# A three-stage attention and MLP kernel: 32x32 block transposes on the vector engine, and weighted sums as 32x64 tiles

## The reference

```python
batch, n_heads, seq, head_dim = (4, 8, 768, 64)
chunk, left_ctx, right_ctx = (32, 16, 8)
...
for c in range(seq // chunk):
    k_full = concatenate([mem_k, k[l_start:r_end]])      # 8 + 56 = 64 rows
    scores = scale * matmul(q_c, k_full.T)
    a = exp(scores - max(scores)); a = a / (sum(a) + 1e-09)
    out[c_start:c_end] = matmul(a, v_full)
...
h = maximum(maximum(x @ w1, x @ w2), x @ w3); x = h @ w_out      # 3072 x 512, d_ff 768
h = x @ w_in; g = where(h >= 1, h, where(h <= -1, 0, (h + 1) ** 2 / 4)); out = g @ w_out   # d_ff 2048
```

## Time and profile before

| what | value |
|---|---|
| median of 3 runs | 988.83 us (988.78 to 989.06) |
| the profiled execution, its own time | 989.49 us |
| its span, first to last instruction | 987.7 us |
| PE busy | 970.1 us (98%), 7968 matmul records |
| DVE busy | 469.3 us (48%) |
| ACT busy | 354.6 us (36%) |
| POOL busy | 150.1 us (15%) |

### The profile page before, as it was taken

How to read it: one execution, slowest core, us unless ns; L and a number is a source line. 1 busy time by engine, 2 the same in 40 slices (tenths; PEclk the granted TensorE clock), 3 DMA queues, 4 the chain that set the end, 5 groups by cost and what they waited for, 6 DMA issues and landing times.

```text
span 987.7 us, 18546 instructions
## 1 busy us (share of the span) xinstructions
PE 970.1 (98%) x7968; PEld 905.5 (92%) x7968; DVE 469.3 (48%) x713; ACT 354.6 (36%) x553; POOL 150.1 (15%) x176
## 2 busy tenths in 40 slices
PE   5999999999999999999999999999999999999998
PEld 4999999999999999999988989899898989888887
DVE  4572514344252433425356655566545665454452
ACT  3341222222122222222344535544455544444253
POOL 1112342315225231000000000000000000000000
PEclk9999999999999999999999999999999999999999
DMA  9452743745464461042635565655657545574532
GB/s 371 174 204 97 261 178 129 251 142 181 176 226 174 167 229 61 1 171 64 248 136 196 204 250 192 224 192 192 240 192 251 189 162 192 189 255 173 194 117 107
DMA packets 32206, 181.52 MB, mean 184 GB/s; under 512 B 3456, under 2 KB 7552, under 8 KB 21888
## 3 DMA queue, kind: packets, MB, share of 16 engines
q0 software_dynamic: 9216, 92.28, 26.7%
q1 hardware_dynamic: 22912, 88.09, 24.2%
HBM read 144.70 MB, written 35.65 MB: 183 GB/s over the span
## 4 chain that ended last, share of the span: by engine, by line
PE 97%; ACT 1%; DVE 1%; DMA 0%; issue 0%
PE mlp L465 23%; PE mlp L466 23%; PE mlp L467 22%; PE attn_ps L467 3%; PE attn_ps L466 3%; PE attn_ps L465 3%; PE scores_ps L467 3%; PE scores_ps L466 3%; PE scores_ps L465 3%; PE attn_ps L458 3%; PE scores_ps L434 2%; PE trans_ps L467 1%; PE trans_ps L466 1%; PE trans_ps L465 1%; PE trans_ps L441 1%; DMA qk_raw<-qk_l 0%
## 5 line engine op out<-in xcount | busy, mean ns | idle before, releaser
L465 PE MATMUL mlp<-x_hi,w_hi 128*128 128x384 f32 x576 | 197.4, 343 | 1.6 <-issue 1.6
L467 PE MATMUL mlp<-x_lo,w_hi 128*128 128x384 f32 x576 | 193.7, 336 | 0.0
L466 PE MATMUL mlp<-x_hi,w_lo 128*128 128x384 f32 x576 | 193.4, 336 | 0.0
L465 PE MATMUL mlp<-yc,wi 128*128 128x384 f32 x448 | 149.6, 334 | 1.5 <-ACT up L628 1.5
L466 PE MATMUL mlp<-yc,wi 128*128 128x384 f32 x448 | 150.8, 337 | 0.0
L467 PE MATMUL mlp<-yc,wi 128*128 128x384 f32 x448 | 149.7, 334 | 0.0
L743 ACT ACTIVATE ramp<-up,half_col 128x768 f32<-128x768 f32 x64 | 60.1, 939 | 197.0 <-DVE up L959 177.9
L465 PEld LDWEIGHTS mlp<-x_hi,w_hi 128*128 128x128 f32 x576 | 108.7, 189 | 3.6 <-issue 1.7
L466 PEld LDWEIGHTS mlp<-x_hi,w_lo 128*128 128x128 f32 x576 | 108.8, 189 | 0.0
L467 PEld LDWEIGHTS mlp<-x_lo,w_hi 128*128 128x128 f32 x576 | 108.7, 189 | 0.0
L465 PEld LDWEIGHTS mlp<-yc,wi 128*128 128x128 f32 x448 | 84.1, 188 | 9.6 <-ACT up L628 1.8
(11 more groups left out here) (111 smaller groups left out, 1643.7 us busy)
## 6 DMA issues: line engine op xcount, KB each, us to landing
wi<-wi_scratch POOLq DMA_DIRECT2D x32, 1792.0 KB, 7.5
wo<-wo_scratch POOLq DMA_DIRECT2D x32, 1024.0 KB, 5.1
qk_raw<-qk_l SPq DMA_DIRECT2D x24, 768.0 KB, 8.3
wi_scratch<-stage_a SPq DMA_DIRECT2D x8, 1792.0 KB, 8.8
v_raw<-v_l SPq DMA_DIRECT2D x24, 512.0 KB, 4.8
wo_scratch<-stage_a SPq DMA_DIRECT2D x8, 1024.0 KB, 6.8
y_scratch<-y_stage SPq DMA_DIRECT2D x32, 192.0 KB, 3.2
y_raw<-y_scratch SPq DMA_DIRECT2D x8, 768.0 KB, 5.5
```

The lines of the kernel that those rows point to most:

```text
L465: pe.matmul(out_ap, a_hi, b_hi, start=first, stop=False, skip_group_check=beside)
L466: pe.matmul(out_ap, a_lo, b_hi, start=False, stop=False, skip_group_check=beside)
L467: return pe.matmul(out_ap, a_hi, b_lo, start=False, stop=last, skip_group_check=beside)
```

## The change

`transposes`, `transposed`, the identity and their semaphores go. A DVE instruction (`dve.transpose`, STREAM_TRANSPOSE) at the end of `softmax_scale` transposes each 32x32 block of the 128x512 probabilities from SBUF to SBUF, into `prob_t`, which now has two buffers. The four chunks of a group stay in their own strips of 32 partitions, so the 64 window rows of a head are two blocks of 32. `weighted_v` therefore contracts 32 rows at a time: 64 matmuls of 32 rows by 64 columns where there were 32, the two halves `x` of a window summed in PSUM, chunk c in row strip c and PSUM bank c. The host lays v and the first weights out to match. The eight PSUM banks become one array: banks 5 to 7 for the products, 0 to 3 for the weighted sums, 0 and 1 for the scores of the passes; in the prologue the three groups' scores have two banks each, and the second group's sums use banks 4 to 7.

In the prologue the three scores come first, then the three sums; DVE does three shifts, three scales with their transposes, then three `x_low`. In the passes `scores(j)` stands ahead of the even block and `weighted_v(j)` where the transposes were; DVE has softmax_scale ahead of `h_second`, and `x_low` in the odd block. ACT has the exponent ahead of `h_first` in the even block and `x_high` after it in the odd one.

The diff, without the semaphore declarations, the padding of one SBUF buffer and the host's layouts:

```diff
@@ -86,11 +86,10 @@
-        v_raw = sbuf(phase_a, "v_raw", [GPT, HALF_HEADS, CPG, D])
+        v_raw = sbuf(phase_a, "v_raw", [GPT, H, 2, D])
...
-        prob_t = sbuf(phase_a, "prob_t", [HALF_HEADS, CPG, CHUNK])
-        ident = sbuf(phase_a, "ident", [P])
+        prob_t = sbuf(phase_a, "prob_t", [2, H, 2, CHUNK])
@@ -128,24 +127,34 @@
-        mlp = [psum(f"mlp{i}", BANK)[:, :] for i in range(3)]
-        attn_ps = psum("attn_ps", 2 * BANK)
-        scores_ps = psum("scores_ps", 2 * BANK)
-        trans_ps = psum("trans_ps", BANK)
+        banks = psum("banks", 8 * BANK)
+        attn_ps, rest_ps = banks[:, 0:4 * BANK], banks[:, 4 * BANK:8 * BANK]
+        mlp = [rest_ps[:, w * BANK:(w + 1) * BANK] for w in range(1, 4)]
...
-        out_acc = (mlp[2], attn_ps[:, 0:BANK], attn_ps[:, BANK:2 * BANK], scores_ps[:, 0:BANK],
-                   scores_ps[:, BANK:2 * BANK], trans_ps[:, :])
-        scores_v = scores_ps[:, :].rearrange("p (r x) -> p r x", r=2)[:, :, 0:HALF_HEADS * WIN].rearrange(
-            "p r (j k) -> p r j k", j=HALF_HEADS)
-        score_v = score[:, :, :].rearrange("p (r j) k -> p r j k", r=2)
+        out_acc = (mlp[2], *(banks[:, i * BANK:(i + 1) * BANK] for i in range(5)))
...
+        def scores_of(n):
...
+            i = 2 * n if isinstance(n, int) and n < GPT else 0
+            return banks[:, i * BANK:(i + 2) * BANK].rearrange("p (r x) -> p r x", r=2)[:, :, 0:HALF_HEADS * WIN].rearrange(
+                "p r (j k) -> p r j k", j=HALF_HEADS)
...
+        def score_of(n):
...
+            return first_of(n) if isinstance(n, int) and n < GPT else score[:, :, :]
...
+        def first_of(n):
+            return y_stage[:, :, :].rearrange("p d t -> p (d t)")[:, n * H * WIN:(n + 1) * H * WIN].rearrange("p (h k) -> p h k", h=H)
...
+        last_e = h_max[:, :, :].rearrange("p i t -> p (i t)")[:, 0:H * WIN].rearrange("p (h k) -> p h k", h=H)
...
-        trans_v = trans_ps[:, :].rearrange("p (m q) -> p m q", m=HALF_HEADS)
-        trans_c = trans_ps[:, :].rearrange("p (m c q) -> p m c q", m=HALF_HEADS, c=CPG)
-        attn_half = attn_ps[:, :].rearrange("p (i x) -> p i x", i=2)[:, :, 0:2 * P]
-        attn_o = attn_half.rearrange("p i (m c q) -> p i m c q", m=2, c=CPG)
-        attn_x = attn_half.rearrange("p i (m q) -> p i m q", m=2)
-        first_e = [mlp[j].rearrange("p (h k) -> p h k", h=H) for j in range(GPT)]
...
+        def sums_of(n):
...
+            ps = rest_ps if isinstance(n, int) and n == 1 else attn_ps
+            return ps.rearrange("p (c x) -> p c x", c=CPG)[:, :, 0:KD * CHUNK].rearrange("p c (k q) -> p c k q", k=KD)
         def q_of(j):
@@ -193,7 +201,7 @@
         def x_of(x, j):
-            return x[:, :, j * P:(j + 1) * P].rearrange("p (m i) q -> p i m q", i=2)
+            return x[:, :, j * P:(j + 1) * P].rearrange("p k (c q) -> p k c q", c=CPG)
         def weights_split(e, n):
@@ -329,11 +337,6 @@
         def _(pool):
-            pool.memset(ident[:, :], 0.0).then_inc(ident_zero, 1)
-            pool.wait_ge(ident_zero, 1)
-            pool.affine_select(out=ident[:, :], in_=ident[:, :], compare_op=ALU.not_equal, fill=1.0, base=0,
-                               pattern=[[-1, P]], channel_multiplier=1).then_inc(ident_done, 1)
@@ -420,43 +423,36 @@
             def scores_ready(n, j, uses):
...
-                if not isinstance(n, int) or n:
-                    pe.wait_ge(sub_done, n)
...
-            def scores(j):
...
-                q, k = q_of(j), k_of(j)
+                if not isinstance(n, int) or n >= GPT:
+                    pe.wait_ge(x_lo_done, n)
...
+            def scores(n, j):
...
+                q, k, s = q_of(j), k_of(j), scores_of(n)
...
-                            last = pe.matmul(scores_v[part, r, i], q[rows, i, part], k[rows, i, c], start=True, stop=True)
+                            last = pe.matmul(s[part, r, i], q[rows, i, part], k[rows, i, c], start=True, stop=True)
...
-            def transposes(n, slot):
...
-                pe.wait_ge(prob_done, n + 1)
-                for m in range(HALF_HEADS):
-                    last = pe.transpose(trans_v[:, m], prob[:, slot, 2 * m:2 * m + 2], ident[:, :])
-                last.then_inc(trans_done, 1)
             def weights_ready(n, j, uses):
...
-                if not isinstance(n, int) or n:
-                    pe.wait_ge(x_lo_done, n)
...
-            def weighted_v(j):
...
-                for m in range(2):
-                    for c in range(CPG):
-                        for r in range(2):
-                            for i in range(2):
-                                rows = slice(i * D, (i + 1) * D)
-                                last = pe.matmul(attn_o[r * D:(r + 1) * D, i, m, c], v_raw[rows, j, 2 * m + r, c],
-                                                 prob_t[rows, 2 * m + r, c], start=True, stop=True)
...
+            def weighted_v(n, j):
...
+                o = sums_of(n)
+                for k in range(KD):
+                    for x in range(2):
+                        for c in range(CPG):
+                            rows = slice(c * CHUNK, (c + 1) * CHUNK)
+                            for r in range(2):
+                                h = 2 * k + r
+                                last = pe.matmul(o[r * D:(r + 1) * D, c, k], v_raw[rows, j, h, x], prob_t[rows, n % 2, h, x],
+                                                 start=x == 0, stop=x == 1)
...
             def three(out_ap, ab, first, last, beside=False):
@@ -506,48 +502,41 @@
-                    def ahead():
+                    def next_scores():
+                        scores_ready(n0 + j + 1, j + 1, t + 1)
...
+                    def next_sums():
...
-                        if j + 1 < GPT:
-                            scores_ready(n0 + j + 1, j + 1, t + 1)
...
-                    if attention and r == 0 and j:
-                        weighted_v(j - 1)
-                        scores(j)
...
-                    layer1(t, a, f, 0)
-                    if attention and f == 0:
-                        scores(0)
+                    if attention and r == 0:
+                        scores(n0 + j, j)
+                    layer1(t, a, f, 0, next_sums if attention and r else None)
...
-                        transposes(n0 + j, (a + 1 + j) % 2)
+                        weighted_v(n0 + j, j)
...
-                    layer1(t, a, f, 2, ahead if attention and r else None)
-                if attention:
-                    weighted_v(GPT - 1)
+                    layer1(t, a, f, 2, next_scores if attention and r and j + 1 < GPT else None)
...
-            pe.wait_ge(ident_done, 1)
-            scores_ready(0, 0, 0)
-            scores(0)
-            scores_ready(1, 1, 0)
-            scores(1)
-            transposes(0, 0)
-            scores_ready(2, 2, 0)
-            scores(2)
-            weights_ready(0, 0, 0)
-            weighted_v(0)
-            transposes(1, 1)
-            weights_ready(1, 1, 0)
-            weighted_v(1)
-            transposes(2, 0)
-            weights_ready(2, 2, 0)
-            weighted_v(2)
+            for j in range(GPT):
+                scores_ready(j, j, 0)
+                scores(j, j)
+            for j in range(GPT):
+                weights_ready(j, j, 0)
+                if j == 0:
...
+                    pe.wait_ge(sub_done, 2)
+                elif j == 1:
+                    pe.wait_ge(sub_done, GPT)
+                else:
+                    pe.wait_ge(x_lo_done, 1)
+                weighted_v(j, j)
@@ -629,28 +618,20 @@
             def exponent(n, slot):
...
-                if not isinstance(n, int) or n >= 2:
-                    act.wait_ge(trans_done, n - 1)
-                act.activation(prob[:, slot], score[:, :, :], ACT.Exp, scale=float(D) ** -0.5).then_inc(exp_done, 1)
+                act.activation(prob[:, slot], score_of(n), ACT.Exp, scale=float(D) ** -0.5).then_inc(exp_done, 1)
             def first_exponent(n):
...
-                act.activation(first_e[n], score[:, :, :], ACT.Exp, scale=float(D) ** -0.5).then_inc(exp_done, 1)
+                e = prob[:, n] if n < 2 else last_e
+                act.activation(e, score_of(n), ACT.Exp, scale=float(D) ** -0.5).then_inc(exp_done, 1)
             def w_high(n):
...
-            def transposed(n):
...
-                act.wait_ge(trans_done, n + 1)
-                if not isinstance(n, int) or n:
-                    act.wait_ge(attn_done, n)
-                copy(prob_t[:, :, :, :], trans_c).then_inc(prob_t_done, 1)
...
             def x_high(n, x, j):
...
-                copy(x_of(x_hi[x], j), attn_x).then_inc(x_hi_done, 1)
+                copy(x_of(x_hi[x], j), sums_of(n).rearrange("p c k q -> p k c q")).then_inc(x_hi_done, 1)
             def h_first(t, a, f):
@@ -674,30 +655,22 @@
-                    if r == 0 and j:
-                        x_high(n0 + j - 1, 1 - a, j - 1)
-                    h_first(t, a, f)
...
-                    else:
-                        transposed(n0 + j)
```

(63 more changed lines are left out.)

12 lines of the change are left out of this document (5 added, 7 removed).

## The result

The changed kernel takes 997.85 us (median of 4 runs, 997.02 to 998.53) against 988.94 us for the kernel before: a ratio of 1.0086, with a 95% interval from 1.0074 to 1.0098. It is slower by 8.9 us. The profiled execution, the fastest of the four, took 997.02 us, 7.53 us more than that of before.

A forecast was written before the change was run, and what follows sets the result against it. PE was taken to bound the kernel; -1.1 (passes) + 0.8 (prologue) + 0.3 (first pass's end) = 0.0 us, so 988.9 us against the median of 988.83. Forecast's own range 987.3 to 992; overall 986 to 1003.

The forecast's parts named there:

- slower: Whole kernel: the case of a time more than 0.2% above the kernel before, chance 0.46.
- B: Sums in the passes: only four places run at once, 30 ns a matmul, interruption 2.2 us, 1003 us in all; chance 0.18.
- The new sums in the passes: PE, seven passes: 64 matmuls a group interrupt for 1.53 us; 0.16 us less a pass, -1.1 us in all.
- A: Sums in the passes: priced at the scores' mean, 24.4 ns a matmul, interruption 1.775 us, 993.9 us in all; chance 0.14.
- The transpose: DVE's transpose in the passes: 0.7 us each, covered with 3.4 us of slack.
- Rival C: DVE's transpose is slow, 1.4 us or more: prologue 2.1 us later, passes still cover it, 991.0 us; chance 0.08.
- The prologue: Before the first pass: DVE's chain starts the third sums at 22.05 instead of 21.23 us, +0.8 us.
- The end of the first pass: First pass, last weight piece: w_low ends at 72.3 with PE ready at 71.95, +0.3 us, once.
- The slow clock: PE's half-rate stretch as the first pass begins: taken as equally long, 0, or 1 us either way.

The follow-up runs named there:

- e4: Changed kernel with the two inner loops of the weighted sums swapped, so the row strip changes at every matmul; 998.55 us, one run.
- e3: Changed kernel, but POOL starts its first weight split only after the third transpose is done; 998.76 us, ratio 1.0099 to the kernel before.
- e1: Changed kernel, but the prologue's three weighted sums do only the first half of each window, 32 matmuls a group instead of 64; 991.64 us, one run.
- e2: Changed kernel, but the fourth weight piece and the q and k loads behind it wait for the third weighted sum; 995.20 us, ratio 1.0061 to the kernel before.
- e7: Changed kernel with DVE's scales ahead of the third shift, POOL's first split behind the third transpose, and later loads held back; 992.81 us, ratio 1.0033 to the kernel before.
- e5: Changed kernel with DVE's prologue reordered: scale 0 ahead of shift 2, scale 1 and the first x_low ahead of scale 2; 996.3 us, one run.

## Why the prediction was right and wrong

The range of 986 to 1003 us holds the result, and slower had 0.46. The forecast itself, no change at 988.9, did not come true, and neither did any rival: none of them was the cause. That the range holds is luck: its upper part stood there for slow sums in the passes (B), and the time was lost in the prologue. Two slips of its arithmetic weigh nothing: 1.52 us is rounded to 1.53, and a burst of 1.65 us gives 991.4 as the forecast's upper end, not 992.

- **The new sums in the passes: right in kind, 0.1 us too small.** Forecast 1.53 us of interruption, measured 1.625. The quick first 32 records came as the scores' burst had shown. The slower rest took 21 ns a matmul, where I had 17 and a gap of 0.08 us. Over 21 bursts this is 2.0 us, and turns -1.1 into +0.95 us. Rival B is refuted: 64 matmuls of 32 rows by 64 columns did not run four at a time. A's price of 1.775 was 0.15 too high. The Trainium skill's rule that no matmul starts within about 25 ns of the one before (TensorE: Matmul & The Clock Gate, "Wait — 56ns, not 53.3ns?") does not agree with 32 records in 0.27 us, nor with a whole burst of 64 matmuls begun in 1.3 us, 20 ns each. Its rule that a weight load overlaps matmuls in flight only when the row group differs (the Trainium skill, same page, Part 3, "The mechanism"), which spoke for B, is not borne out: e4 changes the row strip at every matmul instead of every second, and its burst takes 1.30 us as well.
- **The transpose: right.** 0.71 us, forecast 0.7; no wait for `prob_t` in any pass. Rival C falls.
- **The prologue: the step that failed.** I had +0.8 us, from DVE's chain alone: third sums at 22.05 and the pass at 25.6. It was +6.7. Of the 5.8 us between 25.6 and 31.42, two stalls inside bursts are 5.05. Two things were left out. First, the product's source moved from PSUM to SBUF, and DVE was held by POOL for 1.9 us. e3 shows the hold, and that the second burst goes on at 22.05 with it and without it. Second, and this is the step that cost most, I treated PE's bursts as work that is always at hand. The sentence "the third sums I leave at 1.93 us" took the array's speed for the burst's length, and did not count that the burst had twice the instructions: e1 removed half of them and the stalls vanished, e2 moved a load and the stall shrank by 2.7 us. The trace of before had a sign of it, a gap inside its first weighted sums for which no semaphore accounts, and I read over it. It has the same mark as the others: a piece of instructions began between 12.0 and 12.2 us, its 31.5% of the engines over 0.2 us are 1.0 us, so it landed at 13.1, and PE went on 1.3 us later. The rows are the DMA view of 12.0 to 12.2 us and PE's timeline:

```profile
q8 instruction: 1, 0.02, 31.5%
```

```profile
14.44 1.29 PE L458 MATMUL attn_ps<-prob_t,v_raw 64*64 64x32 f32 x39 [0.15 <-issue]
```

- **The end of the first pass: right in kind.** +0.3 forecast, +0.5 measured.
- **The slow clock: within its bounds.** I took 0 with 1 us either way; it was -0.7. The size is chance: in e4, with the same prologue, the same stretch took 11.83 us (31.43 to 43.26), 0.35 more than before the change.

## What to carry to other kernels

Count instructions, not only engine time, where an unrolled program issues many tiny matmuls in short time: here 64 fp32 matmuls used up one 16 KB piece of instructions in 2 us, and the next piece let PE go on 6.1 us after the last one while loads of data filled the DMA engines (22.1 to 28.2), and 3.3 us after it where they did not (18.4 to 21.7 in e7). Trading 32 matmuls and 4 transposes for 64 matmuls was almost even in array time (0.14 us a pass) and cost 5 us of stalls where the program had just begun and everything was loading at once. When such a stall stands behind a chain, shortening the chain buys little (in e5 1.7 us of 4.3) until the loads are moved as well (e7). And look where a load goes that is held back: in e3 the stall only moved into the pass.

## What the runs showed of the hardware that I had not expected

- Holding loads back made the kernel some 2.5 us faster (e2), because a 16 KB piece of instructions came 2.8 us earlier once no loads of data were under way.
- DVE's product of two SBUF operands took 2.55 us instead of 0.69 while POOL subtracted SBUF operands (15.60 to 19.03 us). With POOL elsewhere it took 0.69 (16.97 to 17.66 in e3), though the DMA engines were as full (a share of 1.06 from 12.5 to 19.5 us, 1.04 in the changed kernel). With one operand in PSUM there was no such hold: in the kernel before, `x_low` ran wholly beside the same POOL work in 0.69 us.

```profile
14.54 3.44 POOL L340 TENSOR_TENSOR w_lo<-stage_a,w_hi 128x1536 fp32r<-128x1536 f32 x1 [13.06 <-ACT w_hi L628]
16.42 0.69 DVE L827 TENSOR_TENSOR x_lo<-attn_ps,x_hi 128x512 fp32r<-128x512 f32 x1
```

- DVE's 32x32 block transpose of 128x512 fp32 took 0.71 us, 0.02 more than a product of the same size.
